# An attention stage and an MLP stage on one NeuronCore, run one after the other or interleaved chunk by chunk

## The chip, the cores and the metric

The kernel runs on 1 core of one Trainium2 chip. The metric is device time in microseconds (us) of that core, as the median of several executions. The profile comes from one more execution, taken with the hardware profiler.

## The reference, cut to what matters

Three layers follow one another. Attention has 4 batches, 8 heads, 768 tokens and head dimension 48; MLP 1 sees 3072 tokens of 384 features; the routed MLP 2 has 8 experts of which each token uses one.

```python
# attention, per batch and head, over tokens t
y[t] = r[t] @ (state + outer(u * k[t], v[t]))
state = w[t][:, None] * state + outer(k[t], v[t])
# MLP 1: w_in 384 x 2048, w_out 2048 x 384
h = x @ w_in
x = maximum(0.01 * h, h) @ w_out
# MLP 2: gate from cosine logits, one expert per token
out[mask] = gate_w[mask, None] * (maximum(x[mask] @ w1[e], 0) @ w2[e])
```

## The kernel before, in words

The work has three stages and a routing step between the second and third.

**Attention** works in 24 chunks of 128 tokens (4 batches of `NCH` = 6), all 8 heads at once, two heads to a group of 128 partitions with each head padded from 48 to 64 rows (`HEAD_PAD`). For a chunk, `turn` (L632) transposes W, R and K through PE (12 transposes). On DVE, `decay` (L1029) and `decay_k` (L1049) scan the decays forwards and backwards and scale R and K. `scores` (L642) makes 8 matmuls of 64 rows, first the four of the upper half of the partitions, then the four of the lower; `mask` (L1071) multiplies by a triangle. `turn_back` (L654) transposes K again. `outputs` (L660) multiplies the decayed R by the state (4 matmuls of 96 columns) and the masked scores by V (8 matmuls of 48 columns), so that tokens are on the partitions; `state_sum` (L678) makes 4 more of 96 columns. Each of these fp32 matmuls is two passes, and so two records, on PE; a transpose is one. The bonus (r times k times u) is made by POOL (`products`, L508), summed by DVE, multiplied with V by POOL and added by DVE in `finish` (L1094), and the result goes to DRAM (`x_attn`). `step` (L689 on PE) works at chunk n on the transposes of n, the scores of n-1 and the outputs of n-2. ACT also loads and splits the weights of MLP 1 during this stage, with POOL making the low parts.

**MLP 1** starts when all of `x_attn` is written (`sp.wait_ge(s_xst...)`). Tokens go in `NG` = 8 groups of 384. Fp32 numbers are held as a high and a low float32r part, so a product is 3 matmuls. For each of 128 steps n = (group g, feature block f of 16), PE makes `feature(n)` (L720, 9 matmuls of 384 columns) and `out_part(n-2)` (L734, 9 more); ACT copies the features out (L926), DVE applies the leaky relu (`leak`, L1176), ACT rounds to the high part (L932), DVE makes the low part (L1181). Each group is loaded from DRAM, transposed on PE (`turn_x`, L711, 9 transposes) and split. DVE also makes the router's products of the group before, 9 for each of 3 token tiles (8 experts and the square norm, L1196).

```python
for n in range(NG * FT + LAG):
    g, f = divmod(n, FT)
    if n < NG * FT:
        feature(n)
        if f == FT // 2 and g + 1 < NG:
            turn_x(g + 1)
    if n >= LAG:
        out_part(n - LAG)
```

Engines run their own instruction streams in order and meet in semaphores: an instruction that waits holds all that is behind it on its engine. **Routing** is a chain of small DVE operations, and **MLP 2** runs the experts' tiles; both stay as they are but for the points named below.

Of the kernel before, what the change touches and what calls it, by code (L numbers as in the profile page):

```python
# [4 lines left out]
F32 = mybir.dt.float32  # L5
F32R = mybir.dt.float32r
I32 = mybir.dt.int32
U32 = mybir.dt.uint32
ALU = mybir.AluOpType
# [9 lines left out]
UP = 1  # L19
LAG = 2  # L20
GS = 4
# [3 lines left out]
def build(nc, r, k, v, w, u, w_in, w_out, emb, tau, w1, w2, out):  # L25
# [13 lines left out]
    NG = TOK // GN  # L39
    MT = (TOK + E * (P - 1)) // P  # L40
    PIECE = 4 * DM
    NW = KT * FF
    NSLOT = 3
    SH = [0, D]
# [6 lines left out]
    with ctx:  # L51
        def sb(name, shape, dt=F32, c=ctx):
            return c.enter_context(nc.sbuf_tensor(name, shape, dt))
# [4 lines left out]
        bank = [ctx.enter_context(nc.psum_tensor(f"bank{i}", [P, 512], F32)) for i in range(8)]  # L58


        WR = sb("WR", [P, 4 * NW], F32R)
        stage = sb("stage", [P, 4, PIECE])
        ident = sb("ident", [P, P])
        tri = sb("tri", [P, P])
        ones = sb("ones", [P, P])
        nbias = sb("nbias", [P, 2])
        viol = sb("viol", [P, B * NCH, 2])
        floor = sb("floor", [P, P])
# [3 lines left out]
        zrow = sb("zrow", [1, DM])  # L72
# [4 lines left out]
        nsq = sb("nsq", [P, NT])  # L77

        s_const = sem("s_const")
        s_bd = sem("s_bd")  # L80
# [3 lines left out]
        s_en = sem("s_en")  # L84


        winh = WR[:, 0:NW].rearrange("p (q k n) -> p q k n", q=4, k=KT)
        winl = WR[:, NW:2 * NW].rearrange("p (q k n) -> p q k n", q=4, k=KT)
        wouth = WR[:, 2 * NW:3 * NW].rearrange("p (f n) -> p f n", f=FT)
        woutl = WR[:, 3 * NW:4 * NW].rearrange("p (f n) -> p f n", f=FT)  # L90

        w_in_p = w_in.rearrange("(k p) (q n) -> q p k n", p=P, q=4)
        w_out_p = w_out.rearrange("(q f p) n -> q p f n", p=P, q=4)

        s_wst = [sem(f"s_wst{i}") for i in range(4)]
# [7 lines left out]

        att = ExitStack()
# [3 lines left out]
        Vn = sb("Vn", [P, NCH, H, D], c=att)  # L108
        Fi = sb("Fi", [P, 2, HP, P + 1], c=att)
        Xi = sb("Xi", [P, HP, P], c=att)  # L110
        Ft = sb("Ft", [P, 2, HP], c=att)
        Rh = sb("Rh", [P, 3, HP, P], c=att)
        Rs = sb("Rs", [P, 2, HP, P], c=att)
        Kh = sb("Kh", [P, 2, HP, P], c=att)
        As = sb("As", [P, 2, 2, HP, P], c=att)
        KhN = sb("KhN", [P, HP, P], c=att)
        St = sb("St", [P, 2, HP, 2 * D], c=att)
        Sm = sb("Sm", [P, HP, 2 * D], c=att)
        Sd = sb("Sd", [P, HP, 2 * D], c=att)
        bd = sb("bd", [P, 2 * D], c=att)  # L120
        rk = sb("rk", [P, H, D], c=att)
        rku = sb("rku", [P, H, D], c=att)
        bonus = sb("bonus", [P, 2, H], c=att)
        Vb = sb("Vb", [P, 3, H, D], c=att)
        ys = sb("ys", [P, 2, H, D], c=att)
        ckj = sb("ckj", [P, H * HEAD_PAD], mybir.dt.bfloat16, c=att)

        s_nat = [sem(f"s_nat{i}") for i in range(NSLOT)]
        s_vin = [sem(f"s_vin{i}") for i in range(NCH)]
# [7 lines left out]
        s_rs = sem("s_rs")  # L137
        s_kh = sem("s_kh")
        s_aA = sem("s_aA")
        s_mk = sem("s_mk")  # L140
# [3 lines left out]
        s_ye = sem("s_ye")  # L144
        s_xst = [sem(f"s_xst{i}") for i in range(2)]
        s_sm = sem("s_sm")
        s_sd = sem("s_sd")
        s_dec = sem("s_dec")
# [4 lines left out]
        s_vb = sem("s_vb")  # L153

        nat = [(Wn, w), (Rn, r), (Kn, k)]

# [3 lines left out]
        block = ctx.enter_context(nc.Block())  # L160

        def before2(b, c):


            n = NCH * b + c - 1
            return max(n, 0) if isinstance(n, int) else n

        def before3(b, c):

            n = NCH * b + c - 2  # L170
            return max(n, 0) if isinstance(n, int) else n

        def nat_val(b, c):

            return 48 * ((NCH // NSLOT) * b + c // NSLOT + 1)

        def ago(b, c, n):

            b, c = (b, c - n) if c >= n else (b - 1, c - n + NCH)
            return None if isinstance(b, int) and not 0 <= b < B else (b, c)  # L180

        def chunks(eng, step, after):

            for c in range(NCH):
                step(0, c)
            with eng.Fori(1, B) as b:
                for c in range(NCH):
                    step(b, c)
            for c in range(after):
                step(B, c)  # L190
# [31 lines left out]
        att.close()  # L222
        q = 4
        DQ = D // q
        gR = sb("gR", [P, TB, D], c=gen)
        gK = sb("gK", [P, TB, D], c=gen)
        gW = sb("gW", [P, TB, D], c=gen)
        gV = sb("gV", [P, TB, DQ], c=gen)
        gY = sb("gY", [P, TB, DQ], c=gen)
        gU = sb("gU", [P, D], c=gen)  # L230
        gS = sb("gS", [P, D, DQ], c=gen)
        gKV = sb("gKV", [P, D, DQ], c=gen)
        gT = sb("gT", [P, D, DQ], c=gen)
        s_gu = sem("s_gu")
        s_gnext = sem("s_gnext")
        s_gin = sem("s_gin")
        s_gy = sem("s_gy")
        s_gst = sem("s_gst")
        s_g = sem("s_g")
        gen.close()  # L240


        m1 = ExitStack()
        xn = sb("xn", [P, GT, DM], c=m1)
        xh = sb("xh", [P, 2, KT, GN], F32R, c=m1)
        xl = sb("xl", [P, 2, KT, GN], F32R, c=m1)
        gt = sb("gt", [P, 2, GN], c=m1)
        gw = sb("gw", [P, 2, GN], c=m1)
        gh = sb("gh", [P, GS, GN], F32R, c=m1)
        gl = sb("gl", [P, GS, GN], F32R, c=m1)  # L250
# [1132 lines left out]
```

## Time and profile before

| | us |
|---|---|
| median of 3 runs (lowest, highest) | 954.49 (953.47, 958.48) |
| the profiled execution's own time | 956.45 |
| its span | 954.5 |
| PE busy | 869.5 (91%) |
| DVE busy | 584.7 (61%) |
| ACT busy | 397.0 (42%) |
| POOL busy | 229.1 (24%) |

The span runs from the first to the last instruction of the profiled execution. Busy times overlap between engines. A line such as L730 is a line of the kernel before. "PEld" is the loading of weights into TensorE, which runs beside its matmuls, and a name with a q (SPq) is an engine's issue of a DMA.

### The profile page before, as it was taken

What the parts mean: (1) busy time and instruction counts of PE and PEld (TensorE: products, weight loads), DVE (VectorE), ACT (ScalarE), POOL (GpSimd) and SP (SyncE); (2) the same over time, 40 slices, a digit from 0 to 9 for tenths busy, and PEclk for the clock granted to TensorE, in tenths of its full rate; (3) what the DMA queues carried; (4) which work ended last, traced back from release to release, by engine and by line L of the source; (5) the groups of instructions that cost most, each with busy time, mean ns of one, the idle gap of its engine ahead of it and who ended that gap; (6) DMA issues with size and microseconds to landing.
All of it is one profiled execution on the core that took longest, in us unless ns stands there. A gap on an engine that the chain in (4) does not pass through costs nothing.

```text
span 954.5 us, 17646 instructions
## 1 busy us (share of the span) xinstructions
PE 869.5 (91%) x5373; PEld 829.5 (87%) x5373; DVE 584.7 (61%) x1334; ACT 397.0 (42%) x760; POOL 229.1 (24%) x283
## 2 busy tenths in 40 slices
PE   5999999879999999999999999505999999999985
PEld 4999898779999999999999999505899899889875
DVE  4899999643465656656565656784425413566875
ACT  3454545323333333233333332231436435576775
POOL 4566767700000000000000000023223323333233
PEclk9999999989999999999999999855999999999999
DMA  9889897360100001010101000002217216377994
GB/s 157 167 148 209 145 209 127 105 249 1 50 1 29 23 1 51 0 51 1 50 1 51 1 25 1 26 2 90 92 42 266 71 43 233 129 283 245 327 322 163
DMA packets 145774, 99.87 MB, mean 105 GB/s; under 512 B 103118, under 2 KB 129909, under 8 KB 145586
## 3 DMA queue, kind: packets, MB, share of 16 engines
q1 hardware_dynamic: 134770, 77.28, 31.0%
q0 software_dynamic: 3776, 10.82, 3.5%
q10 hardware_dynamic: 7168, 11.01, 3.5%
q8 instruction: 32, 0.52, 0.2%
q14 instruction: 28, 0.23, 0.1%
HBM read 132.12 MB, written 14.94 MB: 154 GB/s over the span
## 4 chain that ended last, share of the span: by engine, by line
PE 64%; DVE 6%; DMA 4%; issue 3%; ACT 2%; DVEq 0%; POOL 0%; ACTq 0%; SPq 0%; POOLq 0%
PE bank L744 21%; PE bank L730 21%; PE bank L793 9%; PE bank L819 8%; DMA stage<-in_moe_w_dram 3%; DVE WR L1318 2%; PE bank L805 1%; DVE junk L1196 1%; PE bank L770 1%; ACT WR L961 1%; PE bank L717 1%; DVE vals L1301 1%; PE bank L779 1%; DMA xn<-x_attn 0%; PE bank L673 0%
## 5 line engine op out<-in xcount | busy, mean ns | idle before, releaser
L744 PE MATMUL bank<-WR,gh 128*128 128x384 f32 x768 | 197.5, 338 | 1.7 <-ACT gh L932 1.4
L730 PE MATMUL bank<-xh,WR 128*128 128x384 f32 x768 | 195.8, 337 | 0.0
L1176 DVE SCALAR_TENSOR_TENSOR gw<-gt 128x384 f32<-128x384 f32 x128 | 71.5, 558 | 173.8 <-ACT gt L926 173.6
L926 ACT COPY gt<-bank 128x384 f32<-128x384 f32 x128 | 61.2, 478 | 272.4 <-PE bank L730 272.4
L744 PEld LDWEIGHTS bank<-WR,gh 128*128 128x128 f32 x768 | 139.2, 188 | 2.6 <-ACT gh L932 2.1
L730 PEld LDWEIGHTS bank<-xh,WR 128*128 128x128 f32 x768 | 139.9, 189 | 0.3 <-issue 0.3
L730 PE MATMUL bank<-xl,WR 128*128 128x384 f32 x384 | 130.2, 339 | 0.0
L744 PE MATMUL bank<-WR,gl 128*128 128x384 f32 x384 | 129.3, 337 | 0.0
L819 PE MATMUL bank<-WR,hh 128*128 128x384 f32 x448 | 116.5, 341 | 1.5 <-DVE hl L1346 1.5
L793 PE MATMUL bank<-WR,xgh 128*128 128x512 f32 x336 | 108.5, 405 | 5.4 <-DVE xgl L1333 3.8
L1318 DVE TENSOR_TENSOR WR<-stage,WR 128x1536 fp32r<-128x1536 f32 x58 | 99.7, 1756 | 22.1 <-ACT WR L961 19.4
L568 POOL IOTA desc<- 128x8 f32 x1 | 0.1, 138 | 435.6 <-DVE nsq L1196 435.6
L1196 DVE CUSTOM_DVE_ANT_0 junk<-x2s,embb 128x384 f32<-128x384 f32 x192 | 98.7, 552 | 3.1 <-ACT x2s L920 3.1
L961 ACT CAST WR<-stage 128x1536 fp32r<-128x1536 f32 x60 | 86.9, 1491 | 25.2 <-DMA stage<-in_moe_w_dram 23.0
L819 PEld LDWEIGHTS bank<-WR,hh 128*128 128x128 f32 x448 | 79.3, 188 | 1.8 <-issue 1.8
L793 PEld LDWEIGHTS bank<-WR,xgh 128*128 128x128 f32 x336 | 62.4, 192 | 19.3 <-issue 5.9
L1346 DVE TENSOR_TENSOR hl<-bank,hh 128x512 fp32r<-128x512 f32 x56 | 36.1, 686 | 70.2 <-ACT hh L1006 69.9
L819 PE MATMUL bank<-WR,hl 128*128 128x384 f32 x224 | 75.3, 336 | 0.0
L730 PEld LDWEIGHTS bank<-xl,WR 128*128 128x128 f32 x384 | 72.6, 189 | 0.0
L744 PEld LDWEIGHTS bank<-WR,gl 128*128 128x128 f32 x384 | 72.0, 187 | 0.0
L1181 DVE TENSOR_TENSOR gl<-gw,gh 128x384 fp32r<-128x384 f32 x128 | 70.5, 551 | 0.0
L611 POOL DMA_INDIRECT out_dram<-os,si x28 | 28.6, 1022 | 165.1 <-issue 99.6
(157 smaller groups left out, 1375.9 us busy)
## 6 DMA issues: line engine op xcount, KB each, us to landing
stage<-in_moe_w_dram SPq DMA_DIRECT2D x120, 768.0 KB
Wn<-in_w_dram SPq DMA_DIRECT2D x24, 192.0 KB, 4.1
Rn<-in_r_dram SPq DMA_DIRECT2D x24, 192.0 KB, 4.8
Kn<-in_k_dram SPq DMA_DIRECT2D x24, 192.0 KB, 4.8
Vn<-in_v_dram SPq DMA_DIRECT2D x24, 192.0 KB, 4.0
x_attn<-ys ACTq DMA_DIRECT2D x24, 192.0 KB, 2.9
xn<-x_attn SPq DMA_DIRECT2D x8, 576.0 KB, 4.5
x_moe<-x2s SPq DMA_DIRECT2D x24, 192.0 KB, 2.2
```

The costliest lines, as they stand in the source:

```text
L611: pool.indirect_dma_start(out, bass.IndirectOffsetOnAxis(ap=si[:, s_, 0:1].bitcast(U32), axis=0), os[:, s_, :], None, bounds_check=TOK - 1 ...
L730: mm = pe.matmul(bank[3 + n % 2][:, 0:GN], w_[:, f // 4, k_, cols], a[:, g % 2, k_, :], start=(k_ == 0 and n_ == 0), stop=(k_ == KT - 1 an ...
L744: mm = pe.matmul(bank[5 + i][:, 0:DM], a[:, z, cols], w_[:, f, :], start=(f == 0 and n_ == 0), stop=(f == FT - 1 and n_ == 2))
L793: mm = pe.matmul(bank[3 + a][:], x_[:, k_, :], w_[:, a, k_, :], start=(k_ == 0 and n_ == 0), stop=(k_ == KT - 1 and n_ == 2))
L819: mm = pe.matmul(bank[5 + s_][:, 0:DM], h_[:, f, :], w_[:, f, :], start=(f == 0 and n_ == 0), stop=(f == FT2 - 1 and n_ == 2))
L926: act.copy(gt[:, n % 2, :], bank[3 + n % 2][:, 0:GN]).then_inc(s_g0, 1)
L961: act.copy(dst, src).then_inc(s_ehi, 1)
L1176: dve.scalar_tensor_tensor(gw[:, z, :], gt[:, z, :], 0.01, gt[:, z, :], ALU.mult, ALU.max).then_inc(s_g1, 1)
L1181: dve.tensor_tensor(gl[:, n % GS, :], gw[:, n % 2, :], gh[:, n % GS, :].bitcast(F32), ALU.subtract).then_inc(s_glo, 1)
L1196: dve.tensor_tensor_reduce(junk[:, m % 2, :], x, y, 1.0, 0.0, ALU.mult, ALU.add, to).then_inc(s_lg, 1)
L1318: dve.tensor_tensor(sel(w1l, w2l), src, sel(w1h, w2h).bitcast(F32), ALU.subtract).then_inc(s_elo, 1)
L1346: dve.tensor_tensor(lo, bank[a][:], hi.bitcast(F32), ALU.subtract).then_inc(s_hlo, 1)
```

## The change

The two stages become one. The first three chunks of attention are computed ahead; then chunks 3 to 23 are spread over the steps of MLP 1, three to a group, at fixed steps: for the three chunks of the next group the transposes come at steps 0, 5 and 10, the scores at 2, 7 and 12, the sums at 4, 9 and 13. The sums come out transposed (features on the partitions), as matmuls of 128 columns that write 64 partitions of a bank each: 8 for the state, 8 for the masked scores, and 8 of 64 columns for the new state. The block-diagonal mask goes. The bonus is put on the diagonal of the scores by POOL (a 128x1024 product), and the masked copy is predicated over it. The result is split into high and low straight from PSUM (`y_hi` on ACT, `y_lo` on DVE); the 48-row heads are packed to 384 rows by six small DMAs per group inside SBUF (`fill`), so that `x_attn`, its stores, its loads and `turn_x` go (they are left in a fallback that inputs with out-of-range decays would take). All of the weights of MLP 1 are loaded by SP behind the first three chunks, into a buffer of their own; the router's square norm goes from DVE to ACT (`square`); five POOL iotas go from the routing to the start; the test of `flag` moves from ahead of MLP 1 to behind it; `GS`, the ring of features, goes from 4 to 3.

```diff
+        turn_at, score_at, sum_at = {}, {}, {}
+        for m_ in range(GT, NC):
+            g_, i_ = divmod(m_, GT)
+            turn_at[m_], score_at[m_], sum_at[m_] = [FT * (g_ - 1) + x for x in ((0, 2, 4), (5, 7, 9), (10, 12, 13))[i_]]
...
+            sp.wait_ge(s_const, 1)
+            for m in range(GT):
+                load(m)
+                load_v(m)
...
+            for q_ in range(NQ):
+                load_weights(q_)
+            sp.dma_start(embb[:].rearrange("p e n -> p (e n)"),
...
+            def fill(g):
+
+                sp.wait_ge(s_yhi, GT * (g + 1))
+                sp.wait_ge(s_ylo, GT * (g + 1))
+                for o in range(2):
+                    for k_ in range(KT):
+                        top, from_ = o * HEAD_PAD + D, o * HEAD_PAD + k_ * HOLE
+                        sp.dma_start(xhl[top:top + HOLE, g % 2, :, k_, :].bitcast(F32),
+                                     xhl[from_:from_ + HOLE, g % 2, :, KT, :].bitcast(F32)).then_inc(s_fill, 16)
...
+            for m in range(GT, 2 * GT):
+                next_load(m)
...
+            for n in range(NM + LAG):
+                g, f = divmod(n, FT)
+                for m in at(sum_at, n - 1):
+                    if m + NSLOT < NC:
+                        next_v(m + NSLOT)
+                    if m % GT == GT - 1:
+                        fill(m // GT)
...
+            def diagonal(m):
...
+                pool.tensor_tensor(As[:, m % 2].rearrange("p h o t -> p (h o) t"),
+                                   ident[:].unsqueeze(1).to_broadcast([P, H, P]),
+                                   bonus[:, m % 2, :].unsqueeze(2).to_broadcast([P, H, P]), ALU.mult).then_inc(s_pre, 1)
...
+            def scores(m):
...
                 for h in range(HP):
...
+                    for o, bk in ((0, a_), (1, b_)):
+                        rows = slice(o * HEAD_PAD, (o + 1) * HEAD_PAD)
+                        mm = pe.matmul(bank[bk][:, h * P:(h + 1) * P], Kt[rows, h, :], Rh[rows, m % 2, h, :],
                                        start=True, stop=True)
...
+            def sums(m):
...
+                    for h in range(HP):
+                        for o in range(2):
+                            rows = slice(o * HEAD_PAD, (o + 1) * HEAD_PAD)
+                            pe.matmul(bank[a_][rows, h * P:(h + 1) * P], St[rows, h, :], Rh[rows, z, h, :],
+                                      start=(h == 0), stop=False, skip_group_check=True)
                 for h in range(HP):
                     for o in range(2):
...
+                        rows = slice(o * HEAD_PAD, (o + 1) * HEAD_PAD)
+                        mm = pe.matmul(bank[a_][rows, h * P:(h + 1) * P], Vn[:, s_, 2 * h + o, :], As[:, z, h, o, :],
+                                       start=(m % NCH == 0 and h == 0), stop=True, skip_group_check=True)
...
+                if n < NM and f == 0:
+                    pe.wait_ge(s_fill, 16 * 2 * KT * (g + 1))
...
+                        feature(n)
+                    if not first:
+                        for m in at(sum_at, n):
+                            sums(m)
+                        for m in at(turn_at, n):
+                            turn(m)
+                        for m in at(score_at, n):
+                            scores(m)
...
+            turn(0)
+            turn(1)
+            scores(0)
+            scores(1)
+            sums(0)
+            turn(2)
+            sums(1)
+            scores(2)
+            sums(2)
+            mlp(0)
```

On DVE, step n of the joint stage makes in this order: the low part of the features of n-1, `y_lo` and the state's sum of a chunk summed at n-1, the mask of a chunk scored at n-1, both scans and products (`decay`) of a chunk transposed at n-1, the leaky relu of n, and two router products.

## Rows read from the trace of the kernel before

**Rows 1.** Stages: busy (count) of PE, PEld, DVE, ACT, POOL; clock, DMA share, GB/s.

```profile
30.00:170.00 140.00, 135.51 (x1215) 128.71 (x1214) 128.95 (x314) 73.31 (x184) 100.36 (x94) 1.00 0.90 173
...
197.00:210.00 13.00, 11.46 (x56) 10.72 (x55) 8.54 (x26) 3.82 (x9) 0.00 (x0) 0.87 0.88 320
210.00:606.00 396.00, 396.00 (x2296) 395.77 (x2295) 226.53 (x645) 127.32 (x290) 0.00 (x0) 1.00 0.06 20
```

**Rows 2.** Chain that ended last, 187 to 218: start, us, what.

```profile
187.95 1.87 DMA x_attn<-ys
...
191.18 3.81 DMA xn<-x_attn
...
195.03 2.18 PE bank L717 x9
197.21 4.81 PE bank L730 x18
...
213.44 1.56 PE bank L730 x9
215.00 1.58 PE bank L744 x9
```

**Rows 3.** Timeline of PE, 92 to 102: start, us, what.

```profile
93.29 1.10 PE L684 MATMUL bank<-Vn,KhN 128*128 128x96 f32 x8
94.23 0.60 PE L638 MATMUL bank<-ident,Wn 128*128 128x128 f32 x4
...
95.66 1.68 PE L650 MATMUL bank<-Rs,Kh 64*128 64x128 f32 x16
97.27 1.13 PE L667 MATMUL bank<-St,Rh 128*128 128x96 f32 x8
98.24 1.91 PE L673 MATMUL bank<-Vn,As 128*128 128x48 f32 x16
```

**Rows 4.** PE in slices, line L650 alone: (x) counts the matmuls under way.

```profile
96.40:96.60 0.20, 0.20 (x7) 1.00 1.01 294
...
97.00:97.20 0.20, 0.20 (x4) 1.00 1.22 244
```

**Rows 5.** Groups by line, 210 to 606: busy, mean ns, idle before.

```profile
L1196 DVE CUSTOM_DVE_ANT_0 junk<-x2s,embb 128x384 f32<-128x384 f32 x168 | 87.0, 552 | 0.0
...
L1176 DVE SCALAR_TENSOR_TENSOR gw<-gt 128x384 f32<-128x384 f32 x124 | 69.2, 558 | 170.0 <-ACT gt L926 170.0
```

**Rows 6.** Timeline of the first 32 us, all engines: start, us, what.

```profile
5.86 1.14 SPq L365 DMA_DIRECT2D Rn<-in_r_dram  x1
...
8.84 1.08 PE L638 MATMUL bank<-ident,Wn 128*128 128x128 f32 x4 [8.84 <-DMA Kn<-in_k_dram]
8.89 1.00 POOL L513 TENSOR_TENSOR rk<-Rn,Kn 128x384 f32<-128x384 f32 x1 [3.85 <-DMA Kn<-in_k_dram]
...
16.45 3.09 PE L650 MATMUL bank<-Rs,Kh 64*128 64x128 f32 x16
...
19.23 0.42 SPq L365 DMA_DIRECT2D Wn<-in_w_dram  x1
```

**Rows 7.** Timeline of DVE, 90 to 105: start, us, what.

```profile
96.81 1.36 DVE L1038 TENSOR_TENSOR_SCAN Fi<-bank,floor 128x128 f32<-128x128 f32 x4
...
100.54 0.69 DVE L1063 TENSOR_TENSOR Kh<-bank,Xi 128x512 f32<-128x512 f32 x1 [0.19 <-issue]
101.15 1.28 DVE L1076 TENSOR_TENSOR As<-bank,tri 128x512 f32<-128x512 f32 x2
```

**Rows 8.** Groups by line, 60 to 140, POOL: busy, mean ns, idle before.

```profile
L523 POOL TENSOR_TENSOR Vb<-Vn,bonus 128x384 f32<-128x384 f32 x12 | 9.9, 829 | 22.5 <-DVE bonus L1069 22.5
```

**Rows 9.** DMA issues: line, queue, count, KB each, us to landing.

```profile
Vn<-in_v_dram SPq DMA_DIRECT2D x24, 192.0 KB, 4.0
```

**Rows 10.** Timeline after MLP 1, all engines: start, us, what.

```profile
623.63 0.14 POOL L568 IOTA desc<- 128x8 f32 x1 [435.60 <-DVE nsq L1196]
...
624.94 0.18 DVE L1241 TENSOR_SCALAR rd<-rc 128x24 f32<-128x24 f32 x1 [1.39 <-POOL place L572]
```

More of the change, by code:

```diff
@@ L177, in ago, with states @@
[L177 to L190, printed above, removed]
+        NC = B * NCH
+        def states(m):
+            return m - m // NCH
@@ L574, in _ @@
+            state(NC - 2)
             pool.wait_ge(s_te, 1)
@@ L689, in step @@
-            def step(b, c):
-                now, one, two = (ago(b, c, n) for n in range(3))
-                if now:
-                    turn(b, c, Wn, 0, s_suf, s_wT)
-                    turn(b, c, Rn, 1, s_rh, s_rT)
-                    turn(b, c, Kn, 2, s_kh, s_kT)
-                if one:
-                    scores(*one)
-                if one and one[1] < NCH - 1:
-                    turn_back(*one)
-                if two:
-                    outputs(*two)
-                if one and one[1] < NCH - 1:
-                    state_sum(*one)
@@ L705, in _ @@
-            chunks(pe, step, 2)
-            pe.wait_ge(s_vs, 1)
-            pe.matmul(bank[0][:, 0:1], ones[:], violsum[:], start=True, stop=True).then_inc(s_vt, 1)
+                if more(m):
+                    pe.wait_ge(s_k2n, states(m) + 1)
+                    for h in range(HP):
+                        for o in range(2):
+                            rows = slice(o * HEAD_PAD, (o + 1) * HEAD_PAD)
+                            mm = pe.matmul(bank[b_][rows, h * HEAD_PAD:(h + 1) * HEAD_PAD], KhN[:, h, rows],
+                                           Vn[:, s_, 2 * h + o, :], start=(h == 0), stop=True, skip_group_check=True)
+                    mm.then_inc(s_sm, 1)
@@ new lines, in _ @@
+            act.wait_ge(s_const, 3)
+            check_decays(0)
+            back(0)
+            check_decays(1)
+            back(1)
+            y_hi(0)
+            y_hi(1)
+            split_hi(0)
+            check_decays(2)
+            back(2)
+            split_hi(1)
+            y_hi(2)
+            mlp(0)
+            act.wait_ge(s_flag, 1)
+            f_ = act.value_load(flag[0:1, 0:1], min_val=0, max_val=1)
+            with act.If(f_ > 0):
+                mlp(NM)
+                act.wait_ge(s_sq, 2 * NT)
@@ L1106, in step @@
-            def step(b, c):
-                now, one, two, three = (ago(b, c, n) for n in range(4))
-                if two and two[1] < NCH - 1:
-                    state(*two)
-                if three:
-                    finish(*three)
-                if now:
-                    decay(b, c)
-                    decay_k(b, c)
-                if one:
-                    mask(*one)
-                if now:
-                    bonus_sum(b, c)
-            chunks(dve, step, 3)
-            dve.wait_ge(s_ck, UP + 2 * B * NCH)
@@ L1126, in _ @@
+            bonus_sum(0)
+            decay(0)
+            bonus_sum(1)
+            decay(1)
+            mask(0)
+            mask(1)
+            y_lo(0)
+            state_sum(0)
+            bonus_sum(2)
+            decay(2)
+            y_lo(1)
+            state_sum(1)
+            mask(2)
+            split_lo(0)
+            y_lo(2)
+            state_sum(2)
+            split_lo(1)
+            mlp(0)
             dve.wait_ge(s_flag, 1)
-            f = dve.value_load(flag[0:1, 0:1], min_val=0, max_val=1)
@@ L1128, in _ @@
-            with dve.If(f > 0):
-                for i in range(2):
-                    dve.wait_ge(s_xst[i], UP + 16 * B * NCH // 2)
+            f_ = dve.value_load(flag[0:1, 0:1], min_val=0, max_val=1)
+            with dve.If(f_ > 0):
                 dve.wait_ge(s_gu, 16 * q * B)
@@ L1223, in _ @@
[L1223 removed]
+                mlp(NM)
             done = [0]
```

988 lines of the change are left out of this document (501 added, 487 removed).

## The prediction

> **What bounds the kernel now.** I read the stages first. In the middle of attention PE is busy 135.5 of 140 us, DVE 129.0, so both are close to full; in MLP 1 PE is busy 396.0 of 396.0 and DVE 226.5 [rows 1]. The chain confirms it: in MLP 1 it runs through PE alone, 1.56 us for 9 matmuls and 1.58 us for the other 9 [rows 2], so a step is 3.14 us and 128 steps 402 us. Between the stages the chain leaves PE: from 187.95, when the last attention result goes to DRAM, to 197.21, when the first feature matmul starts, 9.3 us pass, and the first 18 matmuls take 4.81 us where 3.12 would do, as PE is at its lower clock (1.2 GHz) after the idle stretch [rows 2]. At 213.44 the chain is at the features of step 5, so 123 blocks of 1.56 and 125 of 1.58 are to come, and seven `turn_x` of 9 transposes at 0.12 each (Part 2): 213.4 + 389.4 + 7.6 = 610. I predict how this end of MLP 1 moves, then the tail.
>
> The lesson is in what follows: putting work of a stage with PE at 97% between steps of a stage with PE at 100% hides nothing behind PE. It can only win by fewer PE microseconds per chunk, by the gap, and by `turn_x`.
>
> **Part 1: the three chunks ahead.** These are a dependent chain, once. R, W and K are there at 8.84 [rows 6]; loads now wait for four memsets, I take 9.5. Then on DVE: bonus (two POOL products of 1.0 each [rows 6], one sum) to 12.2, `decay(0)` 4.4 (96.81 to the end of the scaled K at 101.23 [rows 7]) to 16.6. POOL makes the diagonal (1024 columns at 829 ns per 384 [rows 8], 2.2 us) and the next two products, so `decay(1)` runs 17.2 to 21.6. PE is cold here: 16 passes took 3.09 us at 16.45 against 1.68 [rows 6, 3]. Scores of 1 (2.9), mask (1.3 [rows 7]) and sums(0) (4) overlap only in part, y_lo and the state's sum end at 31, `turn(2)` and `decay(2)` at 36.6, sums(1) and scores(2) at 41.5, mask and a weight split on DVE at 44.8, sums(2), y_hi and y_lo at 48, fill 4 us later (a landing takes about 4.0 [rows 9]): **52 us**. DMA as a second bound: 12 loads of 192 KB at 173 GB/s (13.6 us), 7.9 MB of weights and router data at the 320 GB/s of 197 to 210 (25 us) [rows 1], from 2.4 us on: 41 us, and 44 us with chunk 3's loads, which stand behind them in SP's queue. At 173 GB/s for all it is 65 us. I take 52, with 44 and 65 as ends. Cold clock at the first steps: +2.
>
> **Part 2: PE time of a chunk between the steps.** From starts of blocks [rows 3]: 12 transposes 1.43 us (94.23 to 95.66), so 0.12 each; scores 1.61 (to 97.27); state product 0.97 (8 passes); masked scores 1.9 (16 passes); new state 0.94 (8 passes). A pass of 48 columns costs as much as one of 128, about 0.11; both load 128 columns of weights, so I take the load as what sets it.
> - Transposes, unchanged: 1.43 x 21 chunks = 30.0.
> - Scores: the same 16 passes, halves alternating. What that may give: where one half is at work, 4 matmuls are under way in 0.2 us; where the first half's last passes meet the second half's first, 7 [rows 4]. So halves of the rows run side by side. Eight pairs at 0.11 are 0.9; with a change of form 1.1. Ends 0.9 and 1.61. 1.1 x 21 = 23.1.
> - Transposes back, 4 x 0.12 = 0.49, for the 17 of 21 chunks that are not a batch's last: 8.3.
> - State product: now 16 passes of 128 columns, each on its own rows and columns of the array. Ends 0.9 (side by side) and 1.8 (one by one); I take 1.1, since its rows are split like the scores'. 18 chunks: 19.8.
> - Masked scores: 16 passes on all rows, only the output columns split. No row shows that; ends 0.9 and 1.8, I take 1.4. x 21 = 29.4.
> - New state, 16 passes of 64 columns: 0.45 to 1.75, I take 0.8, x 17 = 13.6.
> - Changes of form, three more per chunk at 0.1 (16 passes at 0.11 with one overlap should give 1.5, where 1.61 is measured [rows 3]): 6.3.
>
> Sum **130.5 us**, 6.2 per chunk; ends 103 (4.9) and 183 (8.7). Before, the same blocks [rows 3] with the 0.49 make 7.3 for a whole chunk and 6.9 on average over a batch, so PE's own saving is some 14 us over 21 chunks.
>
> The Trainium skill speaks against the state product: "TensorEngine Tiling (Array Packing)", Gotcha 1, says that different row tiles cannot access the same PSUM bank at once, and both halves of `sums` write one bank. By it the product would go one by one, 1.8. The scores write two banks, before as after, so [rows 4] does not decide it; it is in rival B.
>
> **Part 3: waits in the joint stage.** DVE per group: 16 steps of twice 0.56, 24 products at 0.55 [rows 5], 3 chunks of 4.4 + 1.3 [rows 7] and three more operations of 0.55: 53 us; PE 16 x 3.14 + 3 x 6.2 = 69. DVE is not the bound, but order matters. `decay` blocks DVE for 4.4 us from 2.9 us after the features of its step; the scores come 6.3 us (two steps) plus 1.4 (transposes) after those features, so 7.7 against 7.5: hidden by a hair. The features delayed behind it have two steps of slack (their `out_part` is 6.3 us later). The third chunk's sums come one step after its scores: mask done at 13.1, PE there at 12.4: 0.6 us x 7 = 4 us. The turn after a sum waits for y_hi, y_lo and the state sum, about 2.2 us after the sums, while PE has 3.1 us of work: hidden. The ring of features falls from 4 to 3: `feature_hi` of n waits for `out_part` of n-3, which PE ended a step before: free. Moved to other queues: SP issues 6 small fills per group and the V load ahead of them (7 issues of 0.42 [rows 6]), hidden by the two steps 14 and 15 (10.9 us from the sums' start to the next group's features, need 5.2 for sums, y_hi and y_lo, 2.9 for issues and some 2 for the last landing: 10.1). ACT's squares and POOL's diagonals (2.2 us in 21) are covered by their idle time. With 4 us for starts and odd waits: **8 us**, ends 2 and 45.
>
> **Part 4: the tail.** Three square norms leave DVE's last products: 3 x 0.55 = -1.7. The iotas leave the path: POOL started at 623.63 and DVE got on at 624.94 [rows 10], -0.9. The flag test with its jump over a long block now stands on DVE's path: +1.4 (ends 0 and 3), an estimate from SP's same step before: the store landed at 189.82 and the load began at 191.18 [rows 2]. Net -1.2.
>
> **Sum.** 52 + 2 + 402 + 130.5 + 8 = 594.5, against 610: -15.5, with the tail -16.7. The profiled span is 954.5 (its execution 956.45, 2.0 above the median 954.49); on the median: **938**.
>
> **Rivals.**
> - A, the forecast: row halves overlap, columns partly. 925 to 949. Chance 0.42.
> - A+, all pairs overlap fully and little waits: 103 instead of 130.5, 3 instead of 8: about 908 to 922. For it: the 7 under way [rows 4]. Against: nothing shows pairs in columns. 0.13.
> - B, slower: the pairs of `sums` run one by one (one bank, or no overlap by columns). 18 x 0.7 + 21 x 0.4 + 17 x 0.95 = +37 us: 975; with the new state at 0.9 only, 961. It decides from 0.8 us more per chunk. Against: two streams did run side by side [rows 4]. 0.22.
> - C, slower: the fill. Its place is SP's queue at step 15, behind the V load. With 1.14 us per issue as at the start [rows 6] instead of 0.42 (8.0 for seven) and a landing of 4.0 [rows 9], it lands 17.2 us after the sums' start where PE allows 10.9: 6.3 x 7 = 44 us, 982. It decides from 2.4 us over the margin (17 us in all). Against: each fill has 32 short rows, a load has 1,024. 0.12.
> - D, nothing much: the chain ahead takes 60 or more and small waits eat the rest; 948 to 958. 0.11.
>
> **How the numbers follow.** A measurement can tell some 0.5% (4.8 us) from no change. Faster: A x 0.95, A+, a little of D: 0.56. Same: parts of A, D, B: 0.14. Slower: 0.30. The range leaves out a third of A+ and the ends of B and C: 912 to 978; A's own is 925 to 949.
>
> **What would show it.** Right: no idle of PE from about 52 us on; step of 3.14 kept; the 16 passes of each product of `sums` within some 1.1 us; x_attn gone; MLP 1 ends near 594. Wrong: PE idle before `feature` at each group's start released by a fill (C); blocks of `sums` at 1.8 us (B); DVE full and `scores` waiting for the scaled K; a start over 60.

## The result, and the profile after

The changed kernel takes 997.74 us (median of 4 runs, 996.55 to 1000.65) where the kernel before takes 953.98 (4 runs, 951.19 to 958.48): ratio 1.0459, 95% interval 1.0411 to 1.0506. It is slower by 44 us, where 938 was forecast, within 912 to 978.

The page of the changed kernel, from its parts 1 and 2; its span is 994.8 us. PE's busy share falls from 91% to 85%, and in the granted clock there are slices of 7 and 8 within the joint stage, where before MLP 1 had 1.00 from 210 on [rows 1].

```profile
PE 847.8 (85%) x5621; PEld 794.8 (80%) x5621; DVE 630.5 (63%) x1268; ACT 389.9 (39%) x712; POOL 220.4 (22%) x262
...
PEclk9767899999999999999989999965799999999998
```

The page's part 5 has two DVE operations that became slower on average: the low part of the hidden features, `gl` (L1179), in which nothing was changed, takes 734 ns where it took 551 before (its L1181), and the router's product (L1192) 656 where it took 552 [rows 5]. The router's product now writes its scrap output `junk` as bf16 and not as fp32; that isn't what slows it, since 132 of the 144 between 66 and 600 us still take 0.55 us.

The waits of PE in the changed kernel ahead of routing: total us, times, longest. The scaling of K (`Kt`, L1126) is what PE waited for most. Before, PE stood still between attention and MLP 1, for `x_attn` [rows 2], and not between 210 and 606 of MLP 1 [rows 1].

```profile
PE bank L685 <- DVE Kt L1126: 47.9, 23, 6.4
...
PE bank L703 <- POOL St L579: 17.7, 1, 17.7
...
PE bank L744 <- DMA xhl<-xhl: 6.5, 1, 6.5
...
PE bank L703 <- DVE As L1133: 2.6, 5, 0.6
```

**Three stretches.** The first feature matmul starts at 65.01 and the last `out_part` matmul ends at 651.1; before, MLP 1 ended at 610.0. So what lies behind MLP 1 is 343.7 us against 344.5, and all of the loss stands ahead of 651.1: a start of 65.0 and a joint stage of 586.1.

PE's windows, with busy time, instructions and granted clock: the joint stage as a whole, and two stretches behind a stall of 2.38 us at 327.

```profile
core 0: us, PE busy (x), PEclk, DMA share, GB/s
65.00:651.00 586.00, 539.68 (x3858) 0.96 0.21 42
...
331.20:334.20 3.00, 3.00 (x12) 0.50 0.21 42
334.70:338.90 4.20, 4.20 (x26) 1.00 0.61 82
```

In 586 us PE is idle for 46.3 and that is the sum of two rows of waits: 43.7 of the 47.9 for `Kt` (the rest is before 65) and 2.6 for `As`. The stall at 327 is followed by 3 us at a granted clock of 0.50, that is 1.2 GHz, and then 1.00 again.

**The start.** The timeline at 28 to 66, as start, duration, engine, line, [idle before <-releaser].

```profile
35.37 8.66 SPq L362 DMA_DIRECT2D Rn<-in_r_dram  x1
...
51.28 0.99 POOL L560 TENSOR_TENSOR rku<-Rn,Kn 128x384 f32<-128x384 f32 x1 [19.48 <-DMA Kn<-in_k_dram]
...
53.31 0.62 POOL L579 TENSOR_TENSOR St<-Sx,Fi 128x256 f32<-128x256 f32 x1
...
54.07 1.97 PE L703 MATMUL bank<-Rh,St 64*64 64x128 f32 x16 [17.68 <-POOL St L579]
...
59.37 3.98 SPq L417 DMA_DIRECT2D xhl<-xhl  x6
...
65.01 0.69 PE L744 MATMUL bank<-xhl,WRh 128*128 128x384 f32 x1 [6.54 <-DMA xhl<-xhl]
```

POOL makes the products of chunk 3 ahead of the state of chunk 1 (`products(m)` and then `state(m - 2)` in its loop). Chunk 3's R and K stand in SP's queue behind all weights, and SP needs 8.66 us for the issue of R alone and 4.35 for that of K (44.07 to 48.42). So POOL stands still for 19.5 us with a ready sum behind it, and PE for 17.7. The fill is issued at 59.37, and PE waits 6.5 more.

**A chunk in the joint stage.** DVE and POOL at 299 to 307. DVE does `gl` and the scans of `decay` behind the bonus sum; POOL's diagonal (L571) waits for the same sum.

```profile
299.19 0.55 DVE L1092 TENSOR_REDUCE bonus<-rku 128x8 f32<-128x384 f32 x1
...
299.81 1.90 POOL L571 TENSOR_TENSOR As<-ident,bonus 128x1024 f32<-128x1024 f32 x1 [21.63 <-DVE bonus L1092]
...
299.85 2.27 DVE L1179 TENSOR_TENSOR gl<-gw,gh 128x384 fp32r<-128x384 f32 x1
...
301.67 1.33 POOL L560 TENSOR_TENSOR rku<-Rn,Kn 128x384 f32<-128x384 f32 x1
...
302.05 1.35 DVE L1104 TENSOR_TENSOR_SCAN Fi<-bank,floor 128x128 f32<-128x128 f32 x4
...
305.80 0.69 DVE L1126 TENSOR_TENSOR Kt<-bank,Xi 128x512 f32<-128x512 f32 x1
```

`gl` takes 2.27 us, not 0.56, and ends at 302.12, 0.4 us after the diagonal; the scans begin only then, and `Kt` is done at 306.49. PE, which is through with the step's matmuls at 305.80, goes on at 306.64. At the scores of the next chunk the stall is 2.38 us. There a router's product stands ahead of `gl`, and both are slow, the first beside the diagonal and the second beside POOL's next product. DVE and POOL at 318 to 330:

```profile
321.21 2.14 POOL L571 TENSOR_TENSOR As<-ident,bonus 128x1024 f32<-128x1024 f32 x1 [17.12 <-DVE bonus L1092]
...
321.52 2.25 DVE L1192 CUSTOM_DVE_ANT_0 junk<-x2s,embb 128x384 bf16<-128x384 f32 x1
...
323.31 1.33 POOL L560 TENSOR_TENSOR rku<-Rn,Kn 128x384 f32<-128x384 f32 x1
...
323.70 1.36 DVE L1179 TENSOR_TENSOR gl<-gw,gh 128x384 fp32r<-128x384 f32 x1
```

That is 1.70 us for the product and 0.80 for `gl`, 2.5 us in front of the scans. The 21 stalls for `Kt` in the joint stage are of three kinds: seven of 0.8 us, with `gl` at 2.27; twelve of 2.0 to 2.4, with the pair above; and the first two, 6.4 and 3.3 us, where DVE's split of the weights (L1160, two tensors of SBUF too) takes 3.24 us beside the diagonal and 1.76 elsewhere. PE around the stall of 2.38:

```profile
306.64 1.16 PE L685 MATMUL bank<-Rh,Kt 64*128 64x128 f32 x16 [0.84 <-DVE Kt L1126]
...
329.57 1.16 PE L685 MATMUL bank<-Rh,Kt 64*128 64x128 f32 x16 [2.38 <-DVE Kt L1126]
...
331.13 0.67 PE L765 MATMUL bank<-WRh,gh 128*128 128x384 f32 x1
...
334.16 0.47 PE L744 MATMUL bank<-xhl,WRh 128*128 128x384 f32 x1
...
339.14 1.09 PE L703 MATMUL bank<-Rh,St 64*64 64x128 f32 x16
340.17 1.09 PE L708 MATMUL bank<-As,Vn 128*64 128x128 f32 x16
341.09 0.64 PE L716 MATMUL bank<-Vn,KhN 128*64 128x64 f32 x16
341.65 0.44 PE L765 MATMUL bank<-WRh,gh 128*128 128x384 f32 x1
```

The nine `out_part` matmuls from 331.13 on end at 334.16: 3.03 us, where 1.59 is usual. In the same view stand the blocks that were to be priced: 12 transposes 319.40 to 320.62 (1.22, their rows left out), the state product of `sums` 339.14 to 340.17 (1.03), masked scores to 341.09 (0.92), new state to 341.65 (0.56).

### The profile page after: what moved, and what is told of

It is laid out like the page before. It is cut to its first block and busy times, and to the rows that moved or that the text cites. A ratio compares the mean times of both kernels' runs of the same rounds, so it can differ in the third digit from the quotient of the medians.

```text
span 994.8 us, 17463 instructions
## 1 busy us (share of the span) xinstructions
PE 847.8 (85%) x5621; PEld 794.8 (80%) x5621; DVE 630.5 (63%) x1268; ACT 389.9 (39%) x712; POOL 220.4 (22%) x262
## 5 line engine op out<-in xcount | busy, mean ns | idle before, releaser
L744 PE MATMUL bank<-xhl,WRh 128*128 128x384 f32 x768 | 220.0, 341 | 6.5 <-DMA xhl<-xhl 6.5
L744 PEld LDWEIGHTS bank<-xhl,WRh 128*128 128x128 f32 x768 | 142.7, 190 | 6.7 <-DMA xhl<-xhl 6.7
L571 POOL TENSOR_TENSOR As<-ident,bonus 128x1024 f32<-128x1024 f32 x24 | 48.5, 2020 | 418.1 <-DVE bonus L1092 418.1
L765 PE MATMUL bank<-WRh,gh 128*128 128x384 f32 x384 | 139.9, 364 | 0.0
L765 PE MATMUL bank<-WRl,gh 128*128 128x384 f32 x384 | 133.2, 347 | 0.0
L765 PE MATMUL bank<-WRh,gl 128*128 128x384 f32 x384 | 132.7, 346 | 0.0
L744 PE MATMUL bank<-xhl,WRl 128*128 128x384 f32 x384 | 130.6, 340 | 0.0
L1192 DVE CUSTOM_DVE_ANT_0 junk<-x2s,embb 128x384 bf16<-128x384 f32 x192 | 118.3, 656 | 3.1 <-ACT x2s L937 3.1
L1393 DVE TENSOR_TENSOR WRl<-stage,WRh 128x1536 fp32r<-128x1536 f32 x58 | 99.8, 1756 | 23.1 <-ACT WRh L1024 22.8
L1179 DVE TENSOR_TENSOR gl<-gw,gh 128x384 fp32r<-128x384 f32 x128 | 93.9, 734 | 23.6 <-ACT gh L959 21.9
L1024 ACT CAST WRh<-stage 128x1536 fp32r<-128x1536 f32 x60 | 86.6, 1491 | 25.7 <-DMA stage<-in_moe_w_dram 23.2
L865 PE MATMUL bank<-WRh,hh 128*128 128x384 f32 x224 | 77.2, 345 | 1.5 <-DVE hl L1421 1.5
L685 PE MATMUL bank<-Rh,Kt 64*128 64x128 f32 x384 | 34.7, 330 | 47.9 <-DVE Kt L1126 47.9
```

The source lines that it names most:

```text
L571: pool.tensor_tensor(As[:, m % 2].rearrange("p h o t -> p (h o) t"), ident[:].unsqueeze(1).to_broadcast([P, H, P]), bonus[:, m % 2, :].uns ...
L744: mm = pe.matmul(bank[F_BANK[n % 2]][:, 0:GN], win(t_)[:, f // 4, k_, cols], xhl[:, g % 2, a, k_, :], start=(k_ == 0 and n_ == 0), stop=(k ...
L765: mm = pe.matmul(bank[O_BANK[i]][:, 0:DM], a[:, z, cols], wout(t_)[:, f, :], start=(f == 0 and n_ == 0), stop=(f == FT - 1 and n_ == 2))
L865: mm = pe.matmul(bank[5 + s_][:, 0:DM], h_[:, f, :], w_[:, f, :], start=(f == 0 and n_ == 0), stop=(f == FT2 - 1 and n_ == 2))
L1024: act.copy(dst, src).then_inc(s_ehi, 1)
L1179: dve.tensor_tensor(gl[:, n % GS, :], gw[:, n % 2, :], gh[:, n % GS, :].bitcast(F32), ALU.subtract).then_inc(s_glo, 1)
```

## Experiments

Two theories were set against each other first. **P**: the diagonal on POOL holds up DVE operations beside it, this makes `Kt` late, PE stalls, and its clock falls. **O**: DVE's own order is to blame, with the scans behind the low part of the features, and the diagonal is a bystander. The start is a separate question of two queues: in the expectations **Q** is POOL's and **D** is SP's queue of DMAs.

### The diagonal left out

The product of the identity with the bonus isn't made, so the bonus is missing from the output; `As` is zeroed once.

```diff
-                pool.tensor_tensor(As[:, m % 2].rearrange("p h o t -> p (h o) t"),
...
+                pool.sem_inc(s_pre, 1)
```

> The POOL product that puts the bonus on the diagonal is left out (the masked scores' buffer is zeroed once instead), so the bonus term is missing; all else as in the changed kernel. In the profile of the changed kernel a DVE subtraction with both inputs in SBUF (L1179) takes 2.27 us at 299.85 beside this POOL product, where 0.55 is usual, and PE then waits for the scaled K. Theory P (POOL's product blocks DVE): the mean of that subtraction falls from 734 ns to 560, PE's 47.9 us of waits for the scaled K fall by 25 to 35 us, the lower-clock windows of the joint stage (about 51 us) mostly go, time 945 to 965. Theory O (the order on DVE alone: the scans stand behind the low part of the features): the waits stay above 35 us, time within 10 us of 997.7.

Measured: 962.31 us, 1.0096 (1.0062 to 1.0131) of before; the start is as it was (65.27), the joint stage is 35 us shorter, `gl` is at 642 ns, and PE's waits for `Kt` fell from 47.9 to 27.4. So the diagonal matters, but 20.5 us of the waits went where P had said 25 to 35, and `gl` did not come down to 560. The timeline of this run shows why: POOL's next products now start where the diagonal did, and meet the router's product.

```profile
328.93 1.07 POOL L561 TENSOR_TENSOR rku<-Rn,Kn 128x384 f32<-128x384 f32 x1 [19.82 <-DVE bonus L1091]
...
329.06 1.36 DVE L1191 CUSTOM_DVE_ANT_0 junk<-x2s,embb 128x384 bf16<-128x384 f32 x1
```

The collision moved to another instruction of POOL. `gl` behind it takes 1.37 us too, and eleven stalls of 1.5 us remain, while the chunks with no router's product there have none. What had been taken as a property of the diagonal is one of POOL's other products too.

### The diagonal beside the scans

POOL waits until the forward scans of the chunk are done; nothing is left out.

```diff
+                pool.wait_ge(s_scan, m + 1)
                 pool.tensor_tensor(As[:, m % 2].rearrange("p h o t -> p (h o) t"),
```

> POOL makes the same diagonal product but waits for the forward scan of its chunk, so that it runs beside DVE operations that read one input from PSUM; output as the reference. Theory P (POOL's product blocks only DVE operations with both inputs in SBUF): as without the product, mean of L1179 near 560 ns, 945 to 965. If any DVE operation were slowed by POOL, the scans and scalings grow by up to 2 us instead and the time stays at 990 to 1000. Theory O: no change, 990 to 1000.

Measured: 948.84 us, 0.9944 (0.9919 to 0.9968). One wait more makes the kernel 49 us faster than the changed one. `gl` is at 561 ns, the waits for `Kt` at 7.8, the clock of the joint stage at 0.99. The mask is later at times (7.4 us of PE waits for `As`). The diagonal is long done then; the trace has two router's products of 1.36 and 0.97 us instead of 0.55 ahead of five of those six masks, beside POOL's later operations: what is left of the collision. DVE's order is that of the changed kernel, so theory O, which had 990 to 1000 here, is out, and P holds.

### The scans right behind the bonus sum

`decay(m)` moves on DVE from behind `gl` of the next step to the place behind the bonus sum, so that the diagonal meets operations that read PSUM.

```diff
-                        for m in at(turn_at, n - 1):
-                            decay(m)
...
                         for m in at(turn_at, n):
                             bonus_sum(m)
+                            decay(m)
```

> DVE makes the bonus sum and the scans and scalings of a chunk right behind the leaky relu of the step in which PE transposes it, not behind the low part of its features one step's work later. Theory O and theory P agree that it helps, by different sums: the scans start about 1.6 us after the features instead of 2.9, and POOL's diagonal falls beside the scans. PE's waits for the scaled K fall from 47.9 to under 8 us (those of the first three chunks remain), no lower-clock window between 120 and 640, time 925 to 945. If it does nothing, the waits are of another cause.

Measured: 938.76 us, 0.984 (0.9803 to 0.9876). PE's waits for `Kt` are 4.1 us. The timeline of this run, DVE and POOL:

```profile
293.48 1.35 DVE L1104 TENSOR_TENSOR_SCAN Fi<-bank,floor 128x128 f32<-128x128 f32 x4
...
293.64 1.90 POOL L571 TENSOR_TENSOR As<-ident,bonus 128x1024 f32<-128x1024 f32 x1 [16.53 <-DVE bonus L1092]
...
294.97 0.68 DVE L1114 TENSOR_TENSOR Rh<-bank,Fi 128x512 f32<-128x512 f32 x1
```

The diagonal runs from 293.64 to 295.54 beside the scans L1104 and the scaled R (L1114, 0.68 us, as in the changed kernel), and slows neither. Grouped by line and shape for 66 to 600, first the changed kernel and then this run:

```profile
L1192 DVE CUSTOM_DVE_ANT_0 junk<-x2s,embb 128x384 bf16<-128x384 f32 x144 | 94.4, 692 | 0.0
L1179 DVE TENSOR_TENSOR gl<-gw,gh 128x384 fp32r<-128x384 f32 x112 | 85.1, 760 | 19.6 <-ACT gh L959 18.0
...
L571 POOL TENSOR_TENSOR As<-ident,bonus 128x1024 f32<-128x1024 f32 x21 | 42.8, 2037 | 416.6 <-DVE bonus L1092 416.6
...
L1126 DVE TENSOR_TENSOR Kt<-bank,Xi 128x512 f32<-128x512 f32 x21 | 14.5, 692 | 1.9
```

```profile
L1192 DVE CUSTOM_DVE_ANT_0 junk<-x2s,embb 128x384 bf16<-128x384 f32 x181 | 94.9, 563 | 3.1 <-ACT x2s L937 3.1
...
L1179 DVE TENSOR_TENSOR gl<-gw,gh 128x384 fp32r<-128x384 f32 x128 | 71.7, 560 | 24.4 <-ACT gh L959 23.5
...
L571 POOL TENSOR_TENSOR As<-ident,bonus 128x1024 f32<-128x1024 f32 x21 | 39.9, 1898 | 373.6 <-DVE bonus L1092 373.6
...
L1126 DVE TENSOR_TENSOR Kt<-bank,Xi 128x512 f32<-128x512 f32 x21 | 14.5, 692 | 1.9
```

What reads two tensors of SBUF on DVE (`gl`: `gw` and `gh`; the router's product: `x2s` and `embb`) is slower in the changed kernel, and so is POOL's side; what reads one of them from PSUM has the same duration in both. The joint stage of this run, which has as many PE instructions, 3858:

```profile
core 0: us, PE busy (x), PEclk, DMA share, GB/s
66.40:593.30 526.90, 520.92 (x3858) 1.00 0.23 46
```

Against 586.0 us with 539.68 busy at clock 0.96, it is 526.9 with 520.92 busy at 1.00. So the stalls cost 46.3 - 6.0 = 40.3 us of idle PE and 18.8 us of the same instructions done at the lower clock: 59 us together, more than the whole loss. This edit does two things, it takes `gl` and the router's products from POOL's way and it starts the scans earlier; the run with the diagonal beside the scans did the first alone, for the diagonal, and gave 49 of the 59.

### POOL's order at the start

```diff
+                if m > 2 and more(m - 2):
+                    state(m - 2)
                 products(m)
-                if m > 1 and more(m - 2):
-                    state(m - 2)
+                if m == 2:
+                    state(0)
```

> POOL makes the decayed state of chunk m-2 ahead of the r*k products of chunk m (for m > 2). In the changed kernel the state that sums(2) needs stands behind the products of chunk 3, whose loads land at about 51 us behind all weights; PE waits 17.7 us. Theory Q (POOL's order): sums(2) runs at about 39 us, and the first feature at about 45 to 50. But the transposes of chunk 3 stand in PE's queue right behind the first features and still need that load at 51, so the gain is 10 to 14 us: 984 to 988. Theory D (the queue of DMAs is the bound, with the fill behind it): the fill lands no earlier than 60 and the time falls by less than 5.

Measured: 984.65 us, 1.032 (1.0282 to 1.0358). The wait for the state is gone, and the start still is 64.70. The timeline of this run:

```profile
36.45 9.39 SPq L362 DMA_DIRECT2D Rn<-in_r_dram  x1
...
58.70 4.31 SPq L417 DMA_DIRECT2D xhl<-xhl  x6
...
64.69 0.69 PE L746 MATMUL bank<-xhl,WRh 128*128 128x384 f32 x1 [25.36 <-DMA xhl<-xhl]
```

The fill is issued at 58.70, behind loads that hold SP for 9.39 us at one issue: a wait of 25.4 for it has taken the place of the two of 17.7 and 6.5. Behind the wait that was taken away stood another with the same end. The time is within Q's 984 to 988, but by luck: Q had the first feature matmul at 45 to 50, and the 13 us that this run gains all lie in the joint stage (573.1 against 586.1; idle 40.0 against 46.3, busy 533.1 against 539.8), which neither theory had said. The trace shows where from: behind the diagonal POOL now makes the state, 0.62 us by itself, and not a product of 0.99; the second slow operation of the pair, `gl`, takes 0.97 us for 1.36, and the stalls of 2.38 are 1.98.

### SP's order too

In addition SP takes the weights in two halves: those of the first two quarters and chunk 3 to 5's loads with the fill come first, the last two quarters and `embb` after the fill.

```diff
-            for q_ in range(NQ):
-                load_weights(q_)
-            sp.dma_start(embb[:].rearrange("p e n -> p (e n)"),
...
+            load_weights(0)
...
+            next_load(GT)
+            load_weights(1)
+            next_load(GT + 1)
+            next_v(GT)
+            next_load(GT + 2)
+            next_v(GT + 1)
             fill(0)
-            next_v(2 * GT - 1)
+            next_v(GT + 2)
+            load_weights(2)
+            load_weights(3)
...
```

> The changed kernel with POOL's decayed state first (as in e4) and, in SP's queue, the loads of chunks 3 to 5 and the first fill moved ahead of the second half of the weights and of the router's embedding; the rest as changed. With the state alone first, the first feature still came at 64.7 (POOL's wait gone, a wait of 25.4 us for the fill in its place). Theory Q+D (both queues hold the start, one behind the other): the first feature comes at 45 to 50, and the time falls by 15 to 19 us below e4's 984.7, to 966 to 970. Rival (a bandwidth limit: the same bytes must come first anyway): first feature later than 57 and time over 976.

Measured: 970.1 us, 1.0171 (1.0123 to 1.022). The first feature matmul is at 48.16, 16.5 us earlier than with POOL's order alone; the joint stage is 575.5. POOL's order alone left the start where it was; SP's order alone was not run, so whether it needs POOL's is not shown.

### All three orders, and the same again

> The three orders together: DVE's scans early (e3), POOL's state first, SP's loads reordered (e5). If the losses are separate they add: e3's 938.8 less 15 to 19 us, 918 to 925, which would be 3 to 4% below the kernel before. If the early start only moves the wait (the second half of the weights is late for steps 8 and 12), PE waits for WRl or WRh in the first group and the time stays above 930.

Measured: 920.9 us, 0.9652 (0.9606 to 0.9698): the start at 48.49, the joint stage 527.1 as in the run with the early scans. PE's waits in this run:

```profile
PE bank L749 <- DMA xhl<-xhl: 11.0, 1, 11.0
...
PE bank L708 <- DVE As L1138: 4.0, 7, 0.9
PE bank L690 <- DVE Kt L1131: 3.1, 2, 2.9
```

So both causes are real and nearly add up: 59.0 us off for the scans alone and 27.6 for the start's two orders alone make 86.6, and together they gave 76.8. What is missing, 9.8, is near the 10.6 that the two orders gave in the joint stage (586.1 to 575.5), where the early scans leave little to gain.

### One more order of the fill

With all three orders, the fill also moves ahead of V of chunk 4 and the loads of chunk 5.

```diff
-            next_load(GT + 2)
-            next_v(GT + 1)
             fill(0)
+            next_v(GT + 1)
+            next_load(GT + 2)
             next_v(GT + 2)
```

> e6 with the first fill ahead of chunk 5's loads and of the V loads of chunks 4 and 5 in SP's queue. In e6 the low part of chunk 2 is done at 38.5, but the six fills are issued at 42.5 to 46.8, behind four loads, and PE waits 11.0 us for them until 48.5. If SP's queue is what holds the start, the fills are issued from 38.5 on and the first feature comes 3.5 to 4.5 us earlier (44 to 45): 916 to 918. If the bytes already in flight hold them, less than 1 us.

> e6 once more beside e9 on the same chip, as its base: 919 to 923. Both theories of e9 are read against this.

Measured side by side: 917.55 us (915.82 to 923.45), 0.9606 (0.954 to 0.9672), and 921.0 (920.69 to 922.64), 0.963 (0.9576 to 0.9683). The fill is issued at 40.11 instead of 42.19, PE's wait for it is 6.7 instead of 11.5, and the first feature matmul is 3.05 us earlier. The intervals overlap; what the profile shows is an earlier start, a little less than the 3.5 to 4.5 expected, and of the size of the difference of the medians, 3.5.

### The halves one after the other

On top of the early scans, the three loops of `sums` run first over the heads of the upper rows or columns and then over those of the lower, so that neighbours use different halves of the array only where one half's run meets the other's.

```diff
-                    for h in range(HP):
-                        for o in range(2):
+                    for o in range(2):
+                        for h in range(HP):
...
```

> e3 with the matmuls of the sums in another order: first all of the upper 64 output rows, then all of the lower, instead of in turns. Theory H (two passes on different columns of the array run side by side): blocks of 16 passes grow from 0.92 us (masked scores, all rows) and 1.02 (state, split rows) to 1.4 to 1.7 each, and those of 64 columns from 0.57 to 0.8 or more; with 21, 18 and 17 blocks the time grows by 20 to 30 us over e3's 938.8. Rival (a pass with 64 columns of weights is simply half as long, no overlap): blocks unchanged within 0.1 us and the time within 3 us of e3.

Measured: 960.53 us, 1.0039 (1.0014 to 1.0063), 21.8 us more than with the halves in turns. The matmuls of `sums` in turns (the run with the early scans) and apart (this run), from the timelines of PE:

```profile
307.56 1.09 PE L703 MATMUL bank<-Rh,St 64*64 64x128 f32 x16
308.59 1.09 PE L708 MATMUL bank<-As,Vn 128*64 128x128 f32 x16
309.51 0.63 PE L716 MATMUL bank<-Vn,KhN 128*64 128x64 f32 x16
```

```profile
317.77 1.58 PE L703 MATMUL bank<-Rh,St 64*64 64x128 f32 x16
319.27 1.25 PE L708 MATMUL bank<-As,Vn 128*64 128x128 f32 x13
```

The state product takes 1.03 us in turns and 1.50 apart; a chunk's sums, to the next f32r matmul, 2.51 (307.56 to 310.07) and 3.48 (317.77 to 321.25). 0.97 x 21 is 20.4, a little too much as not every chunk has all three products, and PE's busy time in the joint stage rose by 19.8 (521.0 to 540.8) with 5 to 6 us of idle time in both. In turns the passes of a product start in pairs, the two halves 0.01 us apart and a pair every 0.11 us; apart, a half's passes start 0.11 us from each other all the same. Pairs do run side by side, by rows and by columns, and also in one bank.

### The scores one step later

Without any other edit, the scores of a group's first and second chunk go from step 2 and 7 of a group to 3 and 8; the sums stay at 4 and 9. Each triple is the step of a chunk's turn, scores and sums.

```diff
-            turn_at[m_], score_at[m_], sum_at[m_] = [FT * (g_ - 1) + x for x in ((0, 2, 4), (5, 7, 9), (10, 12, 13))[i_]]
+            turn_at[m_], score_at[m_], sum_at[m_] = [FT * (g_ - 1) + x for x in ((0, 3, 4), (5, 8, 9), (10, 12, 13))[i_]]
```

> The changed kernel with the scores of the first two chunks of a group one step later (steps 3 and 8 instead of 2 and 7), nothing else. If PE's waits are latency of DVE's chain and not DVE's throughput, 14 of 21 waits for the scaled K go: from 47.9 us to 15 to 25, lower-clock windows fewer, time 960 to 975. If DVE were short of time as a whole, the waits move to the mask (L1133) and the time stays at 990 to 1000.

Measured: 976.4 us, 1.0214 (1.0169 to 1.0259), just above the 960 to 975 expected: the waits for `Kt` fell to 19.1 us as expected, but those for `As` rose to 13.7, since the mask now has one step to the sums. A step of cover was moved from one wait to the next. Slack alone gives back 21 us; keeping the diagonal from DVE's way gives 49, and with the scans early as well 59.

## Why the prediction was wrong

By its own steps, on the profiled span; its end of MLP 1 was 594.5 and the end was 651.1, 56.6 us more.

- **Baseline**, MLP 1 ends at 610: 610.0. Right.
- **Part 1, the start, 52 (44 to 65): 65.0.** The chain of DVE, PE and POOL was followed chunk by chunk, but the two queues were not read to the end. POOL's `products(3)` ahead of `state(1)` was not in it, though the order stands in the code, and the DMA bound of 44 with chunk 3's loads was taken for a floor rather than for the time at which POOL goes on (51.3). The upper end of 65 took the low rate for everything and is right by accident. +13.0. (That PE was "cold" at 16.45 rests on the doubled durations alone: the trace of the kernel before reads a granted clock of 1.00 there.)
- **Part 1, cold start, 2:** right for what it was: in the run with the early scans the first 13.6 us have clock 0.89, some 1.5 us. But it was thought to be the only cold stretch.
- **Steps, 128 x 3.14 = 402:** a step is 1.58 and 1.59, 3.17, so 405.8. Why each is 0.03 longer was not tried. +3.8.
- **Part 2, attention on PE, 130.5 (103 to 183):** the blocks come to 21 x (1.22 + 1.09 + 0.92) + 17 x (0.41 + 0.56) + 18 x 1.03 = 102.9. That is A+'s 103, but the changes of form are to be added. The ends 103 and 183 don't follow from the list: its low values add up to 100.0 without the changes of form and 106.3 with them, its high ones to 178.4 with them. The changes of form, 6.3 in the sum, took 9.0: from 290.24 to 311.75 the run with the early scans does five steps and a chunk in 21.51 us, where steps and blocks alone make 5 x 3.17 + 1.22 + 1.50 + 2.51 = 21.08; 0.43 x 21 = 9.0. So 112 for 130.5, -18.6. The Trainium skill's rule in "TensorEngine Tiling (Array Packing)", Gotcha 1, that different row tiles cannot use one PSUM bank at once, would have made the state product 1.8; it took 1.03 in turns and 1.50 apart, with the passes of the two halves starting 0.01 us apart into one bank. The trace does not agree with the rule, and rival B, which rested on it in part, did not happen.
- **Part 3, waits, 8 (2 to 45): 46.3**, above its upper end. This is **the step that failed**. "The scores come 7.7 us after the features, `decay` needs 7.5 or less: hidden by a hair" was right with DVE's durations of before, and the durations did not stay. What stands in front of the scans took up to 2.5 us more, because a POOL product was under way: `gl` alone 1.7 more where no router's product stands there, and elsewhere the router's product 1.7 and `gl` 0.8. A margin of 0.2 us was counted as enough, on DVE's durations alone, although the same Part 3 called POOL's 2.2 us "covered by its idle time". They were; DVE's were not. The term that was put at 4, the mask of the third chunk, took 2.6. +38.3.
- **Part 3, its consequence, not in the sum at all:** seven of the twelve stalls of 2.0 to 2.4 us are followed by a stretch at 1.2 GHz, in which nine f32r matmuls take 3.03 us (331.13 to 334.16) where 1.59 is usual, and the first 50 us of the stage have more of them. 18.8 us of PE's busy time in all. Of the sum of busy time of the joint stage some 2 us are left without an account (539.8 less 405.8, 102.9, 9.0, 1.5 and 18.8).
- **Part 4, the tail, -1.2:** 344.5 to 343.7, -0.8. DVE goes on 15.2 us after the last matmul of MLP 1; before it was 15.0. The flag test shows as 3.04 us of issue before L1316, the upper end of the bound (0 to 3).

The sum by these: 13.0 - 0.5 + 3.8 - 18.6 + 38.3 + 18.8 = 54.8 of 56.6.

**The rivals.** A+ had the overlap right and the waits wrong; its 103 leaves out the 9 us of changes of form. B decides from 0.8 us more per chunk; it was 0.9 us less (18.6 / 21). C, a late fill at each group's start, did not happen: after the first one PE never waits for a fill, though its six issues take 3.98 us (0.67 each, not 0.42). But C's form, a short issue behind a long one in SP's queue, is what holds the start at 65. The mechanism that decided, POOL's product in DVE's way, was named by none. The sign "`scores` waiting for the scaled K" stood among the signs of a wrong forecast, with the wrong reason (DVE full): DVE is busy for 63% of the span. "A start over 60" stood there too, and came true.

With the collision and the two orders mended, the same change gives 920.9 and 917.6 us: 17 and 20 us better than the forecast, mostly because attention's blocks on PE came out 18.6 us lower than it had them.

## What to carry to other kernels

When work of one stage is put between the steps of another, price not only each engine's sum but each pair of engines that now runs at the same instant: here a POOL product that starts just ahead of a DVE operation of two SBUF operands held it up for nearly the product's whole length, and the same product beside operations that read PSUM held up none. A margin of tenths of a us on the path to PE is no cover, because a stall there can be paid twice, as idle time and as the lower clock behind it. And where two queues each hold an item that the start needs, mending one of them can show nothing, as POOL's order did here; look for what stands behind the wait before judging the first edit.

## What the runs showed of the hardware

- **DVE and POOL.** A DVE operation on two SBUF tensors that starts 0.04 us behind POOL's product of 1.90 us takes 2.27 us instead of 0.56, about its own time behind what is left of POOL's. One with 1.36 instead of 0.55 stands behind a product of 1.07. Both end 0.4 us after the product. POOL waits as well: its next product took 1.33 instead of 0.99, and a diagonal that starts 0.16 us behind a router's product takes 2.14 instead of 1.90 (321.21). Scans and scaled R, which read PSUM, take 403 and 676 ns beside the diagonal in the run with the early scans, and the scaled K 692 beside the second product; in the changed kernel, without the diagonal beside them, they take 395, 675 and 692. The Trainium skill has this rule, in "SBUF — State Buffer", section "SBUF: two separate sides": a port pair shared by the two engines is an exclusive lock that is held for a whole instruction, and DVE takes it when both inputs are in SBUF. The trace agrees with each part that it can show. Had it been applied in Part 3, it would have named the place.
- **Pairs in one bank.** 16 passes on a quarter of the array each, rows and columns split, take 1.03 us in turns and 1.50 one half after the other; with columns alone split 0.92 in turns, and both halves of each product write one bank. The order in the program decides: in turns, the two halves' passes start 0.01 us apart.
- **The clock.** A stall of 2.38 us in a stage with PE otherwise full is followed by 3 us at 0.50, and seven such stretches lie behind the first 50 us of the joint stage. Not each stall has one: seven of the twelve of 2.0 to 2.4 us do, and none of the seven of 0.8. The run without these stalls has a mean of 1.00.
- **A DMA issue can take 9 us.** SP needed 8.66 and 9.39 us to issue one load of 192 KB while the weights were in flight, and 4.35 for K right behind the first of these; the six loads of R and K of chunks 0 to 2 took 0.57 to 2.15. What stands behind it in the queue waits as long.
- **A pointer as the scan's start value.** Four backward scans of 127 columns with a start value from a tensor took 1.59 us in the changed kernel (L1118). The same four with a constant took 1.35 in the kernel before (L1056), so neither the direction nor the length is the reason; the forward ones of 128 with a constant take 1.35 too.
